# Gathering slot 0 of a routed expert layer: rows loaded from DRAM for seven tiles, one-hot products for two

## What is computed

```python
# x: 1152 x 512, attention output
p = domain_probs / (domain_probs.sum(-1, keepdims=True) + 1e-09)
for e in range(4):                      # dense mixture
    out += p[:, e:e + 1] * (np.maximum(x @ w1[e], 0.0) @ w2[e])
x = out
do_compute = x @ w_skip > 0             # routed layer
xc = x[do_compute]
e_idx = np.argmax(xc @ w_gate, axis=1)
gate_w = softmax(xc @ w_gate)[e_idx]
for e in range(8):
    mask = e_idx == e
    y[mask] = gate_w[mask, None] * (np.maximum(xc[mask] @ u1[e], 0.0) @ u2[e])
out[do_compute] = xc + y
```

## Time and profile before

| | us |
|---|---|
| median of 3 runs | 649.08 (648.16 to 649.21) |
| the profiled execution | 648.53 |
| its span, first to last instruction | 646.9 |
| PE busy in the span | 622.0 |
| DVE busy | 297.4 |
| ACT busy | 246.6 |
| POOL busy | 76.3 |
| mean granted TensorE clock | 0.993 of full speed |

### The profile page before, as it was taken

One profiled execution on the slowest core, in us unless ns is written; L12 is line 12 of the kernel. 1 busy time (PEld: TensorE's weight loads), 2 busy tenths in 40 slices (PEclk: granted clock), 3 DMA queues, 4 the chain that ended last, 5 costly groups with the idle time before them and its releaser, 6 DMA issues.

```text
span 646.9 us, 9656 instructions
## 1 busy us (share of the span) xinstructions
PE 622.0 (96%) x3410; PEld 555.7 (86%) x3411; DVE 297.4 (46%) x784; ACT 246.6 (38%) x518; POOL 76.3 (12%) x119
## 2 busy tenths in 40 slices
PE   5799999999999999999999999999999999999994
PEld 4688989898989898989899998989888888888883
DVE  5765566634412124512124424445567644771770
ACT  4764445522401013301113321312334754862871
POOL 6560000000000000000000001000012321221221
PEclk9899999999999999999999999999999999999998
DMA  8912232304999996310002221042346967692640
GB/s 262 264 54 86 62 97 91 124 1 150 223 262 232 254 241 198 92 61 0 0 0 70 106 100 60 13 136 75 97 158 209 358 216 248 211 360 54 199 129 9
DMA packets 51232, 89.98 MB, mean 139 GB/s; under 512 B 13112, under 2 KB 17720, under 8 KB 51200
## 3 DMA queue, kind: packets, MB, share of 16 engines
q1 hardware_dynamic: 47760, 82.30, 42.8%
q0 software_dynamic: 3440, 7.26, 4.5%
HBM read 63.88 MB, written 27.08 MB: 141 GB/s over the span
## 4 chain that ended last, share of the span: by engine, by line
PE 90%; DMA 2%; ACT 2%; DVE 2%; issue 1%; SPq 1%; POOL 1%; DVEq 0%; POOLq 0%; ACTq 0%
PE ps_y L999 31%; PE ps_h L999 29%; PE ps_y L1073 9%; PE ps_h L1073 9%; PE ps_o L958 2%; PE ps_s L933 2%; PE ps_s L1088 2%; PE ps_s L978 1%; PE ps_t L946 1%; DMA raw<-u 1%; PE ps_o L1053 1%; DMA raw<-w 1%; PE ps_h L1021 1%; PE ps_t L1062 1%; ACT prob L580 1%
## 5 line engine op out<-in xcount | busy, mean ns | idle before, releaser
L626 ACT ACTIVATE ht_hi<-ps_h 128x384 fp32r<-128x384 f32 (+1 forms) x104 | 48.6, 467 | 240.0 <-PE ps_h L999 231.2
L999 PE MATMUL ps_h<-xt_hi,w_hi_a 128*128 128x384 f32 (+1 forms) x400 | 131.1, 328 | 1.2 <-DVE ht_lo L814 1.2
L999 PE MATMUL ps_h<-xt_hi,w_lo_a 128*128 128x384 f32 (+1 forms) x400 | 129.4, 324 | 0.0
L999 PE MATMUL ps_h<-xt_lo,w_hi_a 128*128 128x384 f32 (+1 forms) x400 | 129.4, 323 | 0.0
L999 PE MATMUL ps_y<-w_hi_a,ht_hi 128*128 128x512 f32 x288 | 115.5, 401 | 0.3 <-POOL w_lo_a L451 0.3
L999 PE MATMUL ps_y<-w_hi_a,ht_lo 128*128 128x512 f32 x288 | 112.7, 391 | 0.0
L999 PE MATMUL ps_y<-w_lo_a,ht_hi 128*128 128x512 f32 x288 | 112.4, 390 | 0.0
L814 DVE SCALAR_TENSOR_TENSOR ht_lo<-ps_h,ht_hi 128x384 fp32r<-128x384 f32 (+1 forms) x104 | 54.8, 526 | 118.5 <-ACT ht_hi L626 118.1
L999 PEld LDWEIGHTS ps_h<-xt_hi,w_hi_a 128*128 128x128 f32 x400 | 75.4, 188 | 2.1 <-DVE ht_lo L814 1.8
L999 PEld LDWEIGHTS ps_h<-xt_lo,w_hi_a 128*128 128x128 f32 x400 | 75.4, 188 | 0.4
L999 PEld LDWEIGHTS ps_h<-xt_hi,w_lo_a 128*128 128x128 f32 x400 | 75.3, 188 | 0.0
(11 more groups left out here) (149 smaller groups left out, 836.2 us busy)
## 6 DMA issues: line engine op xcount, KB each, us to landing
raw<-u SPq DMA_DIRECT2D x40, 512.0 KB, 4.6
x_sorted<-xg SPq DMA_DIRECT2D x4, 4112.0 KB, 44.7
raw<-w SPq DMA_DIRECT2D x32, 512.0 KB, 4.6
x<-u SPq DMA_DIRECT2D x24, 512.0 KB, 5.8
vt<-v SPq DMA_DIRECT2D x17, 256.0 KB, 2.9
xg<-x_sorted POOLq DMA_DIRECT2D x12, 257.0 KB
kt<-k SPq DMA_DIRECT2D x8, 384.0 KB, 4.8
x_sorted<-xg SPq DMA_DIRECT2D x1, 2313.0 KB, 43.5
```

The costliest lines, as they stand in the source:

```text
L626: a.activation(ht_hi[:, pos, 0:P * tiles], ps_h[:, pos % 2, 0:P * tiles], ACT.Relu).then_inc(h_hi_done, 1)
L999: ins = mm(dst, hi_lo[l], rhs_hi_lo[r], start=(first and n == 0), stop=(last and n == 2))
```

## The change

Rows of tiles 0 to 6 that belong to slot 0 are no longer taken with one-hot products. After the scatter of tile 6, POOL waits until the first seven scatters have landed, loads the first 128 rows of `x_sorted` into `xg`, and waits for that load (`early_landed`) before it goes on to the scatters of tiles 7 and 8. PE transposes these rows with four products with the identity, which start the sum in `ps_o` (`early_rows`), and signals `early_taken`; POOL waits for that before it loads slot 1's rows into `xg`. Places that belong to tiles 7 and 8 are blank at that time, and blank rows are zero in their 512 columns. Takes 7 and 8 add their rows as before. The order on PE after the last dense product is now: turn, early rows, logits, take 7, rank, count, take 8. DVE makes match 7 after its part of the logits stage of tile 8. The matches in the dense chunk and the wait for `taken` go away, and `in_slot` has two buffers instead of five.

```diff
--- before.py
+++ after.py
@@ -98,10 +98,10 @@
 
 
 
-    TAIL = [("take", 0), ("take", 1), ("route", "turn", NT - 1), ("take", 2), ("route", "logits", NT - 1)]
-    TAIL += [("take", 3), ("take", 4), ("route", "rank", NT - 1), ("count",)]
-    TAIL += [("take", t) for t in range(5, NT)]
-    MATCHES = 5
+    LATE = NT - 2
+    TAIL = [("route", "turn", NT - 1), ("early_rows",), ("route", "logits", NT - 1), ("take", LATE)]
+    TAIL += [("route", "rank", NT - 1), ("count",), ("take", NT - 1)]
+    MATCHES = NT - LATE
 
     EXTRA = [(0, 1), (2,), (3,), (4,), (5,), (6, 7)]
     EXTRA_FIRST = [(), (4,), (5,), (6,), (7,), ()]
@@ -114,9 +114,6 @@
         def put(pos, *what):
             at.setdefault(pos, []).append(("route",) + what)
 
-        if c == CHUNKS - 1:
-            for t in range(MATCHES):
-                at.setdefault(7 + 3 * t, []).append(("match", t))
         if c == 1:
 
             for i in range(KC):
@@ -263,6 +260,7 @@
         rank_ready, dest_ready, before_ready = sem("rank_ready"), sem("dest_ready"), sem("before_ready")
         rows_blank, out_stored, listed = sem("rows_blank"), sem("out_stored"), sem("listed")
         slots_ready = sem("slots_ready")
+        early_landed, early_taken = sem("early_landed"), sem("early_taken")
         xg_landed, first_ids_landed = sem("xg_landed"), sem("first_ids_landed")
         next_ids_kept, own_ids_ready = sem("next_ids_kept"), sem("own_ids_ready")
         xs_ready, xs_hi_done, xs_split = sem("xs_ready"), sem("xs_hi_done"), sem("xs_split")
@@ -456,6 +454,11 @@
                 g.indirect_dma_start(out=x_sorted, out_offset=bass.IndirectOffsetOnAxis(dest[:, t:t + 1], 0),
                                      in_=x[:, t, :], in_offset=None, bounds_check=E2 * LIST - 1,
                                      oob_is_err=False).then_inc(listed, 16)
+                if t == LATE - 1:
+
+                    pool.wait_ge(listed, 16 * LATE)
+                    pool.dma_start(xg[:], x_sorted[0:P, :]).then_inc(early_landed, 16)
+                    pool.wait_ge(early_landed, 16)
 
             nth = pool.alloc_register("nth")
             later = pool.alloc_register("later")
@@ -513,6 +516,7 @@
             pool.reg_mov(later, 1)
             pool.reg_mov(landed_later, 16)
             pool.wait_ge(listed, 16 * NT)
+            pool.wait_ge(early_taken, 1)
             load_rows(row_1)
             pool.dma_start(next_ids[:], x_sorted[0:P, D:D + 2].bitcast(U32)).then_inc(first_ids_landed, 16)
             pool.wait_ge(first_ids_landed, 16)
@@ -784,9 +788,6 @@
 
             def match(t):
 
-                if t >= MATCHES:
-
-                    dve.wait_ge(taken, t - MATCHES + 1)
                 dve.wait_ge(dve_step, steps[0])
                 d.tensor_scalar(in_slot[:, t % MATCHES, :], slot_row[:], dest_f[:, t:t + 1], None,
                                 ALU.is_equal).then_inc(matched, 1)
@@ -797,8 +798,6 @@
                         attention(*what[1:])
                     elif what[0] == "weights":
                         weights_lo(e + what[1], what[2], what[1] // 2)
-                    elif what[0] == "match":
-                        match(what[1])
                     elif what[0] == "route":
                         route(*what[1:])
 
@@ -886,10 +885,9 @@
             weights_lo(E1, KC, 0)
             for what in TAIL:
                 if what[0] == "route":
-                    if what[1] == "rank":
-                        for t in range(MATCHES, NT - 1):
-                            match(t)
                     route(*what[1:])
+                    if what[1] == "logits":
+                        match(LATE)
             match(NT - 1)
 
             dve.wait_ge(rank_ready, NT + 1)
@@ -1045,14 +1043,22 @@
                                 last.then_inc(y_ready, 1)
                             beside(at, Y0 + FC * i + f)
 
+            def early_rows():
+
+                pe.wait_ge(early_landed, 16)
+                for c in range(KC):
+                    last = mm(ps_o[:, P * c:P * c + P], xg[:, P * c:P * c + P], ident[:], start=(c == 0), stop=False)
+                last.then_inc(early_taken, 1)
+
             def take(t):
 
-                pe.wait_ge(matched, t + 1)
+                pe.wait_ge(matched, t - LATE + 1)
 
                 for c in range(KC):
                     last = mm(ps_o[:, P * c:P * c + P], x[:, t, P * c:P * c + P], in_slot[:, t % MATCHES, :],
-                              start=(t == 0 and c == 0), stop=(t == NT - 1 and c == KC - 1))
-                last.then_inc(taken if t < NT - 1 else xs_ready, 1)
+                              start=False, stop=(t == NT - 1 and c == KC - 1))
+                if t == NT - 1:
+                    last.then_inc(xs_ready, 1)
 
             def turn_slot(s):
 
@@ -1119,6 +1125,8 @@
             for what in TAIL:
                 if what[0] == "take":
                     take(what[1])
+                elif what[0] == "early_rows":
+                    early_rows()
                 elif what[0] == "route":
                     route(*what[1:])
                 else:
```

## The result

The changed kernel takes 655.68 us (median of 6, 654.3 to 657.7) against 648.74 for the kernel before beside it: a ratio of 1.0111, 95% interval 1.0093 to 1.0129. It is slower by some 7 us. I had forecast slower, by 4.0 us, with a range up to 655.8; the ratio times 649.08 is 656.3. The way is right, but the loss is 2.9 us larger than forecast and lies just above the range.

What follows compares the result with a forecast made beforehand. The prediction took PE, busy 96% of the span, as the bound, with its queue of takes setting the tail's end. Terms +0.95 + 1.18 - 1.74 = +0.4, plus +3.6 for the clock, gave 653.1 us from 649.08; range 649.0 to 655.8.

Steps and rivals of the forecast that it cites:

- Part 1: PE's takes: 48 of 72 records go, 5.6 us of PE time, but not 5.6 us of path.
- Part 2: Tile 8's turn on PE: starts at 478.20 instead of 478.96, no longer behind takes 0 and 1.
- Part 3: PE waits for the early load before the early rows, so tile 8's logits come later: +0.95 us.
- Part 4: Tile 8's chain: rank now waits behind take 7, so its place is read later: +1.18 us.
- Part 5: From reading tile 8's place to xs_hi: removed takes shorten 3.62 to 1.88 us, -1.74 us.
- Part 6: Later scatters, slot 1's load, DVE weight pieces and weight loads stay covered: costed at nothing.
- rival R4: Another wait, first weights or slots_ready, ends last and the change is neutral; counted with R1, together 0.22.
- Part 7: Emptier PE in the tail lets its clock fall: +3.6 us, the middle between 1.7 and 5.5.
- upper bound: Clock low from the early rows until slot 0's products bring it back: 5.5 us, 1.7 of it in the slot.
- R1: Clock holds, only the sum of parts 2 to 5 counts: 649.5 us; chance 0.22 together with rival R4.
- R2: Early load costs no wait and the clock holds: -1.3 us, 647.8; chance 0.10.
- R3: Low clock holds further into slot 0, or falls together with late weight loads: +7.6 us, 656.7; chance 0.07.

Runs made afterwards that it cites:

- all holes filled: Changed kernel plus unread products in PE's three tail waits (7 before early rows, 11 before take 7, 3 before take 8): 650.88 us, ratio 1.0040 to the kernel before.
- the three profiles: The changed kernel, unedited, profiled three times: 654.30, 655.45 and 657.06 us.
- slot numbers later: Kernel with the early load behind tile 5 and unread products added, DVE's second weight piece moved ahead of the slot numbers: 647.99 us in its profile.
- the load behind tile 5: Changed kernel with the early load behind tile 5's scatter, tiles 6 to 8 taken with one-hot products: 647.25 us, ratio 0.9981 to the kernel before.

## Where the prediction held, and the term that was too small

**Part 1** (5.6 us of PE time are no gain on the path) holds: the products that went gave no gain on the path, and PE's busy time fell by 2.5 us only, since some of those that are left run at the low clock. **Part 2** holds: the turn starts 0.06 us after x.

**Part 3, the load.** The direction and mechanism are as told: PE stands at the early rows until the load lands. Issue to first product was 3.3 us in the profile (477.93 to 481.22), where I had taken 3.2 to the landing; over all seven profiles with this load it was 3.2 to 3.6, so the 2.6 that the prediction gives beside its own figure is too low here; it was issued 0.78 us ahead of x of tile 8 instead of 1.03, and the logits come 1.35 us later instead of 0.95. With all holes filled, where the clock plays no part, it is 1.17.

**Part 4, the new link** was taken at 1.92 us from the routing steps to the place. At a high clock it is 2.00. **Part 5** (1.88 from the place to xs_hi) is 1.94. So up to xs_hi the high-clock sum is off by little: predicted +0.4, measured 10.51 - 9.83 = +0.68.

**Part 6 and rival R4 hold an error.** I had set slot 0's start at xs_hi plus the usual 0.65, and dismissed slots_ready, which comes earlier. What I left out is that PE reads the slot numbers after it. The last row of the slot numbers starts 1.76 to 1.81 us ahead of slot 0's first product in the five kernels that keep their clock and don't wait for xs_hi. With all holes filled slot 0 starts 1.46 us after xs_hi begins, 0.8 later than xs_hi allows, and moving the numbers moved slot 0. Of the 2.0 us that the filled kernel is slower than the kernel before, 0.68 and these 0.8 are accounted for; the other 0.5 is open, with x of tile 8 coming 0.52 us later in its profile. In the kernel before this was hidden, since DVE had the numbers at 485.99 and xs_hi came at 487.96. In the changed kernel at its low clock both end together (numbers at 491.03, slot 0 at 492.95), so it adds next to nothing there; it is what is late next once the clock is mended.

**Part 7, the clock, is the term that was mis-sized**: +3.6 predicted, where the three profiles show about 4.3, 5.9 and 5.9, and it is most of the loss. The fall itself came as told, and for the reason told: filling the holes removes it. Against the kernel with filled holes the three executions of the changed kernel are 3.6, 5.2 and 5.7 us longer from x to slot 1. Against the sum without the clock and without the slot numbers' wait, +0.68, their losses of 5.11, 6.64 and 7.18 leave 4.4, 6.0 and 6.5. A later load is still in these: the early rows start 2.51, 2.46 and 2.99 us after x, against 2.39 with the holes filled. Less that, it is 4.3, 5.9 and 5.9: more low clock (13.7, then 17.1 and 17.1 us) costs more. Two steps failed:

- I took the middle between "one low stretch of 3.4 us" and "low from the early rows on". In all three profiles the clock was low from the early rows or the logits until into slot 0, without a break: 13.7 to 17.1 us. It came back in none before slot 0, so the first bound was never near. Of the upper bound's terms ahead of slot 0 only that of the early rows was partly missing: they lasted 1.26, 1.91 and 1.30 us, against 1.16 at the high clock.
- The upper bound gave slot 0 one low stretch, 1.7 us. From slot 0's to slot 1's first product it is 12.45 before and 13.80, 14.75 and 15.36 in the three profiles: 1.35, 2.3 and 2.9. Slot 0's products start in an already low clock and pay until it is back, at 495.8 to 500.7.

The median of the result, 655.68, is near the second profile. What that one took more than the first, 1.15 us, goes with 1.53 more between x and slot 1. Of the third's 2.76 more, 2.07 lie there, and x of tile 8 was 1.06 later: its prologue was slower.

Of the rivals, R1 (the clock holds) and R2 (faster) fell by the trace. R3 had the right mechanism, a low clock that holds further into slot 0, at the price +7.6; it was given 0.07, and the measured +6.9 lies nearer to it than to the forecast. By the clock's own price, the upper bound of 5.5 was nearest. The chances don't add up either: the forecast's own range begins at 651.0, above the 650.4 up to which a time can't be told from no change, so with R3 it alone gives 0.68 for slower, where the prediction has 0.65, and R1 and R2 leave at most 0.24 for within, where it has 0.27.

The Trainium skill, "TensorE: Matmul & The Clock Gate", section "What's actually happening", says that the rate follows how busy PE has been of late, and gives idleness as what brings the half rate. The trace agrees with the first, and with the second only loosely: the clock fell at 482.1 with 2.58 us of products in 476 to 480 and 0.78 in 480 to 482, the longest pause being 1.8 us. The pause alone doesn't decide: in the kernel with the slot numbers later PE paused for 1.88 us between full stretches (busy 0.21 us in 486 to 488), and the clock stayed at 1.00.

Not settled: why the load's landing after x varies by 0.7 us between executions (it is issued 0.51 to 0.83 us ahead of x, and takes 3.2 to 3.6 us from there), and whether the one execution at 650.5 of the kernel with the load behind tile 5 had a fall in its tail.

## What to carry to other kernels

Products that fill PE's waits are not free to take away: ask, for each stretch that a change thins out, whether PE stays busy enough to keep its clock, and price a fall as everything on PE from there until dense work has brought the clock back, not as one short stretch. Work moved off PE should leave real work in the waits (here two takes in the long hole and the load issued a tile earlier), and where none is left, unread products are worth their place: 4.8 us in one kernel. They have to fill every hole: behind a fall they run at the low clock themselves and delay real work. When a path is shortened, look for numbers that an engine reads before it may start its next loop; in these traces such a read would show only as idle time.

## What the runs showed of the hardware

- The granted clock fell to 0.50 while PE was still doing products now and then, and stayed there for 13.7 to 17.1 us in the changed kernel. The fall follows either of two holes: one of 1.8 to 2.3 us, with 0.85 ahead of the turn, or one of 2.7 us.
- With work before and behind it, a pause of 1.88 us left the clock at 1.00 (slot numbers later), and so did one of 1.49 us (all holes filled).
- 21 added products of 128x128 made the kernel 4.8 us faster.
- A load of 257 KB from DRAM by POOL took 3.2 to 3.6 us from issue until PE went on.
- PE's first product of a loop whose bounds are read from memory came 1.76 to 1.81 us after the start of the DVE row that wrote them in five kernels, and 2.11 in one.
